# Tokens scattered into one bucket per expert, the first token tile taken from the first three tiles alone, two first tiles written out

## The reference

```python
attn = softmax(mask(q @ k.T / 8)) @ v         # 8 heads of 64; 4 local (32 back), 4 strided by 32
logits = x @ w_gate + modality_bias[modality_id]      # 8 experts
e_idx = np.argmax(logits, axis=1)
h = np.maximum(x[mask] @ w1[e], 0.0)                  # 512 -> 1024, the token's one expert
out[mask] = gate_w[mask, None] * (h @ w2[e])          # 1024 -> 512
out += p[:, e:e + 1] * (relu(x @ w1[e]) @ w2[e])      # dense layer, all 4 experts for every token
```

## Time and profile before

| | |
|---|---|
| Median of 3 runs | 649.45 us (648.29 to 650.33) |
| The profiled execution | 647.75 us |
| Its span | 645.7 us |
| TensorE busy | 611.2 us, 95% |
| VectorE busy | 354.1 us, 55% |
| ScalarE busy | 207.0 us, 32% |
| GpSimd busy | 301.3 us, 47% |
| Mean granted TensorE clock | 0.986 of full speed |
| HBM read, written | 48.70 MB, 5.00 MB |

### The profile page before, as it was taken

One profiled execution on the slowest core, in us unless ns is written; L12 is line 12 of the kernel. 1 busy time (PEld: TensorE's weight loads), 2 busy tenths in 40 slices (PEclk: granted clock), 3 DMA queues, 4 the chain that ended last, 5 costly groups with the idle time before them and its releaser, 6 DMA issues.

```text
span 645.7 us, 10625 instructions
## 1 busy us (share of the span) xinstructions
PE 611.2 (95%) x3665; PEld 535.3 (83%) x3666; DVE 354.1 (55%) x687; ACT 207.0 (32%) x529; POOL 301.3 (47%) x280
## 2 busy tenths in 40 slices
PE   5999667999999999999999999999999999999995
PEld 4888655678876788989988988998998998998894
DVE  5887726852248522368455455545545555545653
ACT  3865306642246422213212312311321321231230
POOL 6543371016000000662999685576576568557005
PEclk9999697999999999999999999999999999999999
DMA  9917153784105201100211110120110111010003
GB/s 231 232 23 261 62 192 133 279 300 157 51 16 213 81 16 32 40 27 1 66 66 65 66 36 32 65 65 2 65 65 16 49 65 32 32 65 0 0 0 147
DMA packets 25650, 54.05 MB, mean 84 GB/s; under 512 B 6680, under 2 KB 9368, under 8 KB 25624
## 3 DMA queue, kind: packets, MB, share of 16 engines
q1 hardware_dynamic: 16904, 28.78, 14.3%
q0 software_dynamic: 6848, 21.52, 9.6%
q10 hardware_dynamic: 1872, 3.41, 1.7%
HBM read 48.70 MB, written 5.00 MB: 83 GB/s over the span
## 4 chain that ended last, share of the span: by engine, by line
PE 79%; issue 5%; DVE 5%; POOL 3%; SPq 3%; ACT 1%; ACTq 1%; DMA 1%; another core or an unknown queue 0%; DVEq 0%; POOLq 0%
PE bank L1267 29%; PE bank L1238 28%; PE bank L1194 8%; PE bank L1206 7%; PE bank L1178 1%; POOL out L516 1%; DVE w_lo L895 1%; SPq L322 1%; PE bank L1072 1%; DMA dprob<-in_moe_domain_probs 1%; DVE w_lo L901 1%; PE bank L1125 1%; ACT w_hi L564 1%; PE bank L1093 1%; PE bank L1172 1%
## 5 line engine op out<-in xcount | busy, mean ns | idle before, releaser
L978 DVE SCALAR_TENSOR_TENSOR acc<-bank,meta_s,acc 128x512 f32<-128x512 f32 x135 | 100.8, 748 | 62.2 <-PE bank L1267 62.1
L1267 PE MATMUL bank<-u_hi,h_hi 128*128 128x512 f32 x288 | 112.2, 390 | 0.0
L1267 PE MATMUL bank<-u_lo,h_hi 128*128 128x512 f32 x288 | 112.1, 389 | 0.0
L1267 PE MATMUL bank<-u_hi,h_lo 128*128 128x512 f32 x288 | 112.0, 389 | 0.0
L465 POOL CAST u_hi<-u_raw 128x1792 fp32r<-128x1792 f32 (+1 forms) x16 | 25.6, 1598 | 107.3 <-PE bank L1238 102.8
L1025 DVE SCALAR_TENSOR_TENSOR h_lo<-bank,h_hi 128x288 fp32r<-128x288 f32 x112 | 50.9, 454 | 44.7 <-ACT h_hi L662 23.0
L1238 PE MATMUL bank<-x2T_hi,u_hi 128*128 128x288 f32 x232 | 68.4, 295 | 0.0
L1238 PE MATMUL bank<-x2T_lo,u_hi 128*128 128x288 f32 x232 | 68.4, 295 | 0.0
L1238 PE MATMUL bank<-x2T_hi,u_lo 128*128 128x288 f32 x232 | 68.3, 295 | 0.0
L1238 PE MATMUL bank<-t_hi,u_hi 128*128 128x288 f32 x224 | 66.2, 295 | 0.0
L1238 PE MATMUL bank<-t_lo,u_hi 128*128 128x288 f32 x224 | 66.0, 295 | 0.0
(11 more groups left out here) (194 smaller groups left out, 1256.3 us busy)
## 6 DMA issues: line engine op xcount, KB each, us to landing
w_raw<-in_moe_w SPq DMA_DIRECT2D x10, 2048.0 KB, 8.2
u_raw<-in_moe_w POOLq DMA_DIRECT2D x16, 512.0 KB, 3.7
u_raw<-in_moe_w POOLq DMA_DIRECT2D x16, 256.0 KB, 3.1
u_raw<-in_moe_w POOLq DMA_DIRECT2D x32, 128.0 KB, 2.8
x_tile<-x_by_rank ACTq DMA_DIRECT2D x13, 256.0 KB
qT<-in_qT SPq DMA_DIRECT2D x4, 576.0 KB, 8.3
kT<-in_kT SPq DMA_DIRECT2D x8, 288.0 KB, 10.1
v_rows<-in_v_by_position SPq DMA_DIRECT2D x12, 128.0 KB, 10.9
```

The costliest lines, as they stand in the source:

```text
L978: w.scalar_tensor_tensor(out=acc[:, t, :], in0=bank[Z_BANK[i]][:], scalar=meta_s[:, t, bass.ds(e + 1, 1)], in1=acc[:, t, :], op0=ALU.mult, ...
L1267: last = t_.matmul(bank[Z_BANK[i]][:], lhs[:, c, ts], rhs[page][:, c, :], start=c == 0 and k == 0, stop=c == 1 and k == 2)
```

## The change

- Every expert gets its own bucket of 1280 rows in HBM (`x_by_expert`); a token goes to its expert's bucket at its rank there, so a place doesn't depend on the other experts' counts. The nine tiles of tokens are scattered in three groups of three. Experts and ranks of the first two groups are found inside attention, those of the last behind it.
- The first run is that of the expert with most tokens in the first group, chosen in step 13 of attention (`choose_first`). Token tile 0 is the first 128 of these; `in_slot` and its 72 matmuls go. SP stores zeros behind the expert's rows and loads tile 0, then w2; later tile 1, then stores zeros behind the rows of each of the eight experts, then loads tile 2.
- w1 of the first run is cut in the last four iterations of attention.
- Tiles 0 and 1 are straight code on TensorE, ScalarE and VectorE, with the cuts of w2 and the making of the table between their pieces; the loops begin with tile 2. A table row says in which tile a run's w2 is cut.
- `flip_rows` for tiles 1 to 3 comes earlier. Buffers are placed anew, so that the ones loaded early don't lie over attention's.
- GpSimd issues the scatter of tile 0 ahead of the last normalisation, of tiles 1 and 2 behind it, and the others when tile 0 is loaded and their group's slots are known. The first weights of the dense layer still wait for tile 2 (the count is 3, since no zeroed result is counted any more).

The core of the diff (buffers, the reworded table, `find_slots`, `count_tiles`, `place_tiles` and `find_meta`, which are some 35 small VectorE steps, are left out; `ROWS` is 1280, `second_layer` and `whole_tile` are the loop's old body as functions):

```diff
+    GROUPS = ((0, 3), (3, 6), (6, 9))
     FLIP_AT, step = {}, 2 * STRIDED - 3
     for t in range(NT):
-        step = max(step + (2 if t < NT // 2 else 1), steps_before(t))
+        step = max(step + (2 if t == 3 else 1), steps_before(t) + (1 if t < 3 else 0))
         FLIP_AT[step] = t
     LOGITS_AT = {step + 1: t for step, t in FLIP_AT.items() if step + 1 < STEPS}
-    FIRST_AT = min(LOGITS_AT) + 2
     FLIP_END = [t for step, t in FLIP_AT.items() if step >= STEPS]
     LOGITS_END = [t for t in range(NT) if t not in LOGITS_AT.values()]
-    MAXT = N // P + E - 1
+    FOUND_AT = {max(step for step, t in LOGITS_AT.items() if t < b): g for g, (a, b) in enumerate(GROUPS[:2])}
+    RANK_AT = {step + 2: g for step, g in FOUND_AT.items()}
+    CHOSEN_AT = min(RANK_AT)
+    W1_AT = [STEPS + LAG_V - 4 + c for c in range(4)]
+    assert GROUPS[2][1] == NT and all(t >= GROUPS[1][1] for t in LOGITS_END) and max(RANK_AT) < STEPS
+    EARLY = 2
+    MAXT = N // P + E + EARLY
...
             sp.wait_ge(first_known, 1)
             expert = sp.value_load(first_expert[0:1, 0:1], min_val=0, max_val=E - 1)
             sp.dma_start(w1_raw[:].unsqueeze(1),
                          w1[bass.ds(expert, 1)].rearrange("e (c p) f -> p e c f", p=P)).then_inc(w1_in, 16)
+            sp.wait_ge(x_first_known, 1)
+            x0 = sp.value_load(x_first[0:1, 0:1], min_val=0, max_val=(E - 1) * ROWS)
+            sp.wait_ge(zero_set, 1)
+            tail = sp.value_load(x_first[0:1, 3:4], min_val=0, max_val=(E - 1) * ROWS + N)
+            sp.dma_start(xb[bass.ds(tail, P), :], zero_row[:]).then_inc(filled_a, 16)
+            sp.wait_ge(filled_a, 16)
+            sp.wait_ge(scattered_a, 16 * GROUPS[0][1])
+            sp.dma_start(x_tile[:], xb[bass.ds(x0, P), :]).then_inc(xt_in, 16)
             sp.dma_start(w2_raw[:].unsqueeze(1),
                          w2[bass.ds(expert, 1)].rearrange("e (c p) d -> p e c d", p=P)).then_inc(w2_in, 16)
+            x1 = sp.value_load(x_first[0:1, 1:2], min_val=0, max_val=(E - 1) * ROWS + P)
+            sp.wait_ge(fill_known, 1)
+            tail = sp.value_load(fill_at[0:1, bass.ds(expert, 1)], min_val=0, max_val=(E - 1) * ROWS + N)
+            sp.dma_start(xb[bass.ds(tail, P), :], zero_row[:]).then_inc(filled_a, 16)
+            sp.wait_ge(filled_a, 32)
+            sp.wait_ge(scattered, 16 * (NT - GROUPS[0][1]))
+            sp.wait_ge(xt_flipped, 1)
+            sp.dma_start(x_tile[:], xb[bass.ds(x1, P), :]).then_inc(xt_in, 16)
+            sp.wait_ge(rest_known, 1)
+            for e in range(E):
+                tail = sp.value_load(fill_rest[0:1, e:e + 1], min_val=0, max_val=E * ROWS)
+                sp.dma_start(xb[bass.ds(tail, P), :], zero_row[:]).then_inc(filled, 16)
+            sp.wait_ge(x2_known, 1)
+            x2 = sp.value_load(x_first[0:1, 2:3], min_val=0, max_val=(E - 1) * ROWS + 2 * P)
+            sp.wait_ge(filled, 16 * E)
+            sp.wait_ge(xt_flipped, 2)
+            sp.dma_start(x_tile[:], xb[bass.ds(x2, P), :]).then_inc(xt_in, 16)
             sp.wait_ge(table_ready, 1)
             n_runs = sp.value_load(table[0:1, 4, 0:1], min_val=1, max_val=E)
@@ -352,11 +399,9 @@
                 with sp.Fori(1, n_runs) as r:
                     expert = sp.value_load(table[0:1, 0, bass.ds(r, 1)], min_val=0, max_val=E - 1)
                     sp.wait_ge(w1_split, r * WCH)
-                    sp.wait_ge(scattered, 16 * NT)
                     sp.dma_start(w1_raw[:].unsqueeze(1),
                                  w1[bass.ds(expert, 1)].rearrange("e (c p) f -> p e c f", p=P)).then_inc(w1_in, 16)
                     sp.wait_ge(w2_split, r * WCH)
-                    sp.wait_ge(xt_in, 16)
                     sp.dma_start(w2_raw[:].unsqueeze(1),
                                  w2[bass.ds(expert, 1)].rearrange("e (c p) d -> p e c d", p=P)).then_inc(w2_in, 16)
...
+            def scatter(t):
+                pool.indirect_dma_start(out=xb, out_offset=bass.IndirectOffsetOnAxis(ap=slot[:, t:t + 1], axis=0),
+                                        in_=xtok[:, t, :], in_offset=None)                    .then_inc(scattered_a if t < GROUPS[0][1] else scattered, 16)
             for i in range(STEPS):
                 R, C, s = rows(i % TILES), keys(i % TILES), i % PB
                 pool.wait_ge(inv_known, i + 1)
                 g.tensor_tensor(prob[0:R, s, :, 0:C], prob[0:R, s, :, 0:C],
                                 row_inv[0:R, s, :].unsqueeze(2).to_broadcast([R, HALF_H, C]),
                                 ALU.mult).then_inc(normed, 1)
-            pool.wait_ge(slot_ready, 1)
-            pool.wait_ge(x_kept_a, (NT + 1) // 2)
-            pool.wait_ge(x_kept_v, NT // 2)
-            for t in range(NT):
-                pool.indirect_dma_start(out=xs, out_offset=bass.IndirectOffsetOnAxis(ap=pos[:, t:t + 1], axis=0),
-                                        in_=xtok[:, t, :], in_offset=None).then_inc(scattered, 16)
-            pool.wait_ge(meta_ready, 2)
+                if i == STEPS - 2:
+                    pool.wait_ge(slot_ready, 1)
+                    pool.wait_ge(x_kept_a, 2)
+                    pool.wait_ge(x_kept_v, 1)
+                    scatter(0)
+            for t in range(1, NT):
+                for g_, (t0, t1) in enumerate(GROUPS):
+                    if t == t0:
+                        pool.wait_ge(xt_in, 16)
+                        pool.wait_ge(slot_ready, g_ + 1)
+                        pool.wait_ge(x_kept_a, (t1 + 1) // 2)
+                        pool.wait_ge(x_kept_v, t1 // 2)
...
+                if i in W1_AT:
+                    act.wait_ge(w1_in, 16)
+                    cut_w1(W1_AT.index(i))
...
             keep_xt(0)
-            act.wait_ge(scattered, 16 * NT)
-            act.wait_ge(zero_out, 16)
-            load_x(1)
+            for t in FLIP_END:
+                if t % 2 == 0:
+                    keep_rows(t)
+            act.wait_ge(w2_in, 16)
+            cut_w2(0)
+            cut_w2(1)
+            keep_h(0, 0)
+            cut_w2(2)
+            act.wait_ge(lmax_known, 1)
+            a.activation(lexp[:], lexp[:], ACT.Exp).then_inc(lexp_done, 1)
+            keep_ht(0, 0)
+            cut_w2(3)
+            keep_h(0, 1)
+            keep_ht(0, 1)
+            keep_xt(1)
+            keep_h(1, 0)
+            act.wait_ge(y_flipped, 1)
+            a.copy(x2T_hi[:, :, 0:P], bank[6][:].rearrange("p (c t) -> p c t", c=DC)).then_inc(x2_hi_kept, 1)
+            keep_ht(1, 0)
+            keep_h(1, 1)
+            keep_xt(2)
+            act.wait_ge(table_ready, 1)
+            act.wait_ge(filled, 16 * E)
+            load_x(3)
...
+            def choose_first():
+                dve.wait_ge(vstep, st.value)
+                step(w.reduce_max(choice[:, 0:1], count_a[:], axis=AX.X))
+                step(w.scalar_tensor_tensor(out=early_n[:], in0=count_a[:], scalar=choice[:, 0:1], in1=e_down[:],
+                                            op0=ALU.is_ge, op1=ALU.mult))
+                step(w.reduce_max(choice[:, 1:2], early_n[:], axis=AX.X))
+                w.tensor_scalar(first_expert[:], choice[:, 1:2], -1.0, float(E), ALU.mult, ALU.add).then_inc(first_known, 1)
+                step(w.tensor_scalar(is_e0[:], e_down[:], choice[:, 1:2], None, ALU.is_equal))
+            def put_in_order():
+                w.tensor_scalar(choice[:, 2:3], choice[:, 1:2], -float(ROWS), float(E * ROWS), ALU.mult, ALU.add).then_inc(vstep, 1)
+                st.next()
+                step(w.tensor_scalar(choice[:, 3:4], choice[:, 0:1], float(P), None, ALU.min))
+                w.tensor_copy(x_first[:, 0:1], choice[:, 2:3]).then_inc(vstep, 1)
+                st.next()
+                w.tensor_tensor(x_first[:, 3:4], choice[:, 2:3], choice[:, 0:1], ALU.add).then_inc(vstep, 1)
+                st.next()
+                step(w.tensor_tensor(x_first[:, 1:2], choice[:, 2:3], choice[:, 3:4], ALU.add))
+                w.tensor_scalar(at_least[:], is_e0[:], float(EARLY), None, ALU.mult).then_inc(x_first_known, 1)
+                w.tensor_scalar(early_n[:], is_e0[:], choice[:, 3:4], None, ALU.mult).then_inc(vstep, 1)
+                st.next()
+                step(w.tensor_tensor(order_tmp[:, 0, :], is_e0[:], run_no[:], ALU.mult))
+                step(w.tensor_tensor(order_tmp[:, 1, :], run_no[:], order_tmp[:, 0, :], ALU.subtract))
                 step(w.tensor_tensor(earlier[:], order_tmp[:, 1, :].unsqueeze(2).to_broadcast([P, E, E]),
                                      order_tmp[:, 1, :].unsqueeze(1).to_broadcast([P, E, E]), ALU.is_gt))
...
+                if m in FOUND_AT:
                     dve.wait_ge(vstep, st.value)
-                    find_experts(slice(0, 1), onehot0_ready)
+                    find_experts(slice(*GROUPS[FOUND_AT[m]]))
+                if m == CHOSEN_AT:
+                    choose_first()
+                if m == CHOSEN_AT + 1:
+                    put_in_order()
+                    find_slots(slice(*GROUPS[0]))
```

(66 more changed lines are left out.)

495 lines of the change are left out of this document (263 added, 232 removed).

## The result

| | before | after |
|---|---|---|
| Median of 17 runs each, one chip | 649.45 us | 651.86 us (650.14 to 652.98) |
| Ratio, 95% interval | | 1.0044 (1.0026 to 1.0062) |
| Profiled span | 645.7 us | 650.9 us |
| Mean granted TensorE clock | 0.986 | 0.967 |

The forecast was 639.5 us. The changed kernel is 0.4% slower. The gather is gone and the first expert matmul does come earlier, at 81.02 us (88.22 before), but the dense layer starts at 265.15 where it started at 260.82: within the routed experts 4.3 us were lost where 9.9 were to be won.

What follows compares the result with a forecast made beforehand. It took TensorE's waits between attention and tile 0's end (43.3 us) as the target. Tile 2 at 110.9, plus 2.0 loop entry and 138.0 tiles, gave 250.9 against 260.82: 9.9 less, 639.5 us, range 632.0 to 648.5.

Steps and rivals of the forecast that it cites:

- A: End of attention: VectorE's added steps cost 3.0 us (bounds 0 and 4.4); last normalisation at 64.45, last flip but one at 72.1.
- B: Way to tile 0: a chain of DMAs replaces the gather; first expert matmul at 76.9 instead of 88.22, gain 11.3 us.
- slower rival: SP's fills take 2.06 us each; TensorE waits before tile 2 and restarts at half speed; 653.4 us, chance 0.07.
- E: SP's eight zero fills before tile 2's load take 8.5 us; rows at 104.2, TensorE waits 3.2 us.
- C: Tile 0: w2 lands at 79.6, tile done at 90.0; 13.1 us instead of 23.3.
- D: Tile 1: rows load only after all scatters land, at 92.0; TensorE waits 2.0 us, first matmul at 94.6.
- F: Entering the loop at tile 2: ScalarE's prologue and first pass cost 2.0 us, bounds 0 and 5.
- G: Tiles 2 to 11: still twelve tiles and five runs, in order 5, 1, 1, 1, 4; 138.0 us.
- fetch of the loop's code in a rival: ScalarE's loop crosses a fetch boundary, so ten passes each pay the first pass's 2.24 us wait: 662 us, chance 0.04.

Runs made afterwards that it cites:

- c4: c3 without its unread matmuls, against the kernel before on a fifth chip, without the stall: 641.51 us, 0.9960.
- c1: Kernel after with run order and bases behind the routing, ScalarE's copy ahead of the table, unread matmuls in three TensorE waits: 645.69 us, 0.9966 of before.
- e5: Kernel after with ScalarE in tile 1 copying the second half of h's high parts before waiting for the table and loading tile 3: 647.63 us, 0.9998 of before.
- e8: Kernel after with GpSimd's nine scatters of positions and gates held until the end of tile 2, on a chip with the stall: 648.69 us, one run.
- e9: Kernel after with SP's loads of the second run's w1 and w2 held until the end of tile 2, on a chip with the stall: 652.26 us, one run.
- b1: Kernel before with its nine scatters of token data held back until tile 5 is kept: 649.33 us, 1.0101 of before.
- c3: Kernel after with c1's edits, w1 splits one iteration later, unread matmuls in five waits, four of eight fills on ScalarE: 640.57 us, 0.9845 of before.
- c2: c1 plus w1 splits one iteration later, more unread matmuls, four fills on GpSimd, scatters of positions behind tile 2: 645.44 us, 1.0024 of before.
- e3: Kernel after with four run-order steps and find_bases moved out of attention into VectorE's wait for the last ranks: 641.30 us, 0.9973 of before.
- a0_again: Kernel after, unchanged, on the second chip, with the stall: 650.11 us, 1.0028 of before.
- a0_third: Kernel after, unchanged, on the third chip, without the stall: 643.76 us, 0.9992 of before.

## Why the prediction was wrong

By its own steps, against the first profile after:

- **A held.** The last normalisation was forecast for 64.45 and began at 64.19, the last flip but one for 72.1 and began at 71.34. What A left out was where the delay of VectorE's longer queue would fall: a wait of TensorE of 2.19 us in one piece, for the 20th normalisation.
- **B failed, by its clock.** The chain of DMAs was right: the load of tile 0 was issued at 69.67 (forecast 70.2 for the scatters' landing) and TensorE found the tile there. But the logits, flips and transposes between 71.34 and 81.02 were priced at full clock and ran at half: the 16 logit matmuls of tiles 7 and 8 took 3.21 us, where B had 1.7 for them. First expert matmul 81.02 instead of 76.9. The half clock had a place in the forecast only in the slower rival, behind the fills. That was the mistake: a wait of 2 us was taken into account as 2 us wherever else it appeared. That the clock is the cause is borne out by c4, which with the other edits, but no unread matmul, kept its clock at full to 72 us and started its first expert matmul at 75.14. (B's own pieces add up to 76.4, not 76.9, and E's to 103.9, not 104.2: with these slips mended the forecast would have been 0.8 us lower and further off.)
- **C** had w2 in time, as forecast. Tile 0's first half took 4.75 us instead of 2.72. From first matmul to first matmul tile 0 took 18.5 us, 17.7 forecast.
- **D held in its terms.** Slots to last landing was forecast as 7.4 us (81.2 to 88.6) and took 7.5 (86.85 to 94.34); the load landed in 2.51; 3.1 was forecast. TensorE waited 2.05 (2.0). Tile 1 began at 99.56 instead of 94.6, the delay of B handed on and 0.8 more. The estimate of 2.6 us from the Trainium skill (DMA: Bandwidth & Descriptors, Anatomy of one DMA), whose fit is for GpSimd's path, was nearer to this load on SP than the row of the store that the forecast took.
- **E: the price was right, the wait didn't come.** Eight fills took 8.00 us (forecast 8.5), one landed in 2.0. But tile 1's first half ran at half clock, 5.49 us instead of 2.72, and so tile 2's rows were there. Where c1 keeps the clock up, the wait is there: 2.09 us, forecast 3.2.
- **F failed in its place.** The loss at the loop was put at its entry. It came before: `place_tiles`, 14 steps on VectorE (109.02 to 113.19), then the load's registers on ScalarE, held `keep_ht(1, 1)` and so TensorE for 2.45 us, and the half clock behind it made 12 matmuls of the second layer take 4.61 us. Where e5 takes that wait away, 2.36 us of it stand at the entry: the price of 2.0 was near, its place and the clock behind it were not foreseen. With E's wait absent and this one in, tile 1 took 20.2 us, 18.3 forecast for it with the entry.
- **G failed in tile 2, the largest single loss, and held in the rest.** Tiles 3 to 11 took 124.4 us (140.80 to 265.15), where 138.0 less one tile of 12.8 makes 125.2. Tile 2 took 21.0 us instead of 12.8. The stall behind it was seen in the earlier trace rows as 2.24 us on an unknown queue, priced only within F, and taken for a fetch of the loop's code in a rival. e8 and e9 show that it goes with GpSimd's scatters of positions, and e8 shows it without any fetch. The kernel before has more of it than that row: the scatters of positions went out from 88.18 to 99.24, and from 92 us on ScalarE's small steps took some 0.7 us each. From the chain of the kernel before:

```profile
92.08 0.69 ACTq L600
...
98.42 0.70 ACTq L592
```

So F's 5.0 us of prologue were in part already this stall; in b1, without these scatters there and on a chip without the stall, the same stretch took 2.75 us (91.28 to 94.03). Why it is 7.29 us in one piece in the kernel after isn't shown: four scatters are issued behind the load there, and seven were before.

The sum: 4.1 (A and B) + 0.8 (C and D) + 1.9 (E and F) + 7.4 (G) = 14.2 us, which is 265.15 less the 250.9 forecast: half of it is the clock and the waits, the other half the stall in tile 2.

Of the rivals none names the cause. SP's fills took 1.0 us each and not 2.06, and the passes behind the first show no refetch; what is right in the slower one is the restart at half speed, which it priced at 2.9 us at one place.

**How much is which.** On chips with the stall the kernel before took 648.6 to 649.9 us and the one after 650.1 and 651.9; on the third chip, without it, 644.3 and 643.8. So the stall costs the kernel after 6 to 8 us (in the profiles tile 2 takes 21.0 us with it and 12.9 without) and, if the medians of before (643.5 to 644.3 on the other chips) are read in the same way, the one before some 5; these are estimates across chips. With it out of both, the change is worth nothing that can be measured (0.9992, 0.9967 to 1.0017), not the 9.9 us forecast: clock and waits have taken all of it. The combination c3 has the same scatters and chain of DMAs, with half of the fills on ScalarE, seven steps and the splits of w1 moved on VectorE, ScalarE's copy ahead of the table and the unread matmuls. Its medians lie 9.3 us below those of before on a chip with the stall and 8.4 on one without; without the unread matmuls (c4) 2.8 of the 8.4 are left. So a kernel with the change can be that much faster, once waits of TensorE of one to two and a half microseconds are shortened or filled. How much of it is the change's own isn't shown, since the kernel before wasn't given unread matmuls, and part of its stages ran at half clock too.

Not settled: why only some chips show the stall, what the held ScalarE waits for inside (the trace calls it remote), what sets off the fall of the clock where a wait is short, and what stopped GpSimd for 3.49 us in c2. Each chip was used in one stretch of runs, so chip and occasion aren't told apart, and the kernel after was run unchanged for the first profile and on the second and third chip of the experiments only.

## What to carry to other kernels

A wait of TensorE of one to two microseconds can cost more than its length, since what follows may run at half clock (2.19 us of waiting were followed by over 20 us of it): cost every piece behind such a wait at both clocks, and where the wait can't be removed, try unread matmuls in it. When TensorE has been made to wait less, read again what the slow clock had hidden; here it was the fills. And move work on a shared helper engine only with a look at what stands behind it in its queue: putting the scatters out of the way cost 4 to 8 us at a later change of weights.

## What was not expected of the hardware

- The same wait of 1.34 us at the same place left the clock at full in c4 (1.00 in the ten microseconds behind it) and was followed by the fall in e3 (0.61 from 62 to 64, then 0.50). So the length of the one wait does not decide it; the two runs were on different chips and differ in VectorE's splits and the fills.
- Chips differ by a stall of ScalarE: with the kernel after unchanged, 21.0, 21.0 and 12.9 us for tile 2 in the first profile, in a0_again and in a0_third.
- On the chips with the stall ScalarE can stand still while GpSimd issues indirect DMAs: 7.29 us behind its own load in the kernel after, 3.11 and 3.93 us ahead of it in e5. No fetch of code ran in the held stretches of the kernel after and of e8.
- VectorE's four splits of a weight took 7.63 us beside GpSimd's cutting of another and 4.63 without.
